# Cluster ties through a triangular matmul, and a new order of loads, moves and lots ahead of the first attention head

## The reference, cut to what matters

```python
def _attn_ref(q, k, v, centroids):                 # q, k, v: 2 x 8 x 768 x 64; centroids: 8 x 16 x 64
    scale = 1.0 / np.sqrt(D)
    q_n, k_n, c_n = ...                            # each row over its norm + 1e-06
    q_assign = np.argmax(np.einsum('bhsd,hcd->bhsc', q_n, c_n), axis=-1)
    k_assign = np.argmax(np.einsum('bhsd,hcd->bhsc', k_n, c_n), axis=-1)
    mask = q_assign[:, :, :, None] == k_assign[:, :, None, :]
    scores = scale * np.matmul(q, k.transpose(0, 1, 3, 2))
    scores = np.where(mask, scores, -1000000000.0)
    scores = scores - np.max(scores, axis=-1, keepdims=True)
    attn = np.exp(scores)
    attn = attn / (np.sum(attn, axis=-1, keepdims=True) + 1e-09)
    return np.matmul(attn, v).astype(np.float32)
...
x = attention, 1536 tokens x 512
h = x @ w_in;   x = (h / (1 + exp(-1.702 * h))) @ w_out              # 512 -> 2048 -> 512
h = x @ w_in2;  s = h * softmax(h)                                   # 512 -> 1024
out = ((s - mean(s)) / sqrt(var(s) + 1e-06) * g_ln) @ w_out2         # 1024 -> 512
```

## Time and profile before

| | |
|---|---|
| median of 3 runs | 666.93 us |
| the profiled execution, its own time | 669.46 us |
| its span, first to last instruction | 667.6 us |
| PE busy | 630.4 us, 94% |
| DVE, POOL, ACT busy | 471.6, 451.9, 354.4 us |
| first matmul of the scores of turn 0 | 34.29 us |
| first `turn` | 46.62 us |
| first matmul of the scores of turn 1 | 61.80 us |

### The profile page before, as it was taken

How to read it: one execution, slowest core, us unless ns; L and a number is a source line. 1 busy time by engine, 2 the same in 40 slices (tenths; PEclk the granted TensorE clock), 3 DMA queues, 4 the chain that set the end, 5 groups by cost and what they waited for, 6 DMA issues and landing times.

```text
span 667.6 us, 11191 instructions
## 1 busy us (share of the span) xinstructions
PE 630.4 (94%) x3245; PEld 529.9 (79%) x3245; DVE 471.6 (71%) x805; ACT 354.4 (53%) x705; POOL 451.9 (68%) x588
## 2 busy tenths in 40 slices
PE   4478999999999999999999999999999999999998
PEld 1267888988989898888878888878888888788876
DVE  3668999999999995564645684855457478778660
ACT  1258989999999985333325344443332144443241
POOL 2667697887988877766675777776666776867100
PEclk9969999999999999999999999999999999999999
DMA  8775545445545340222222222222220000000001
GB/s 279 199 228 138 145 106 144 129 110 143 137 106 145 91 172 32 94 94 96 94 95 94 92 93 97 94 94 93 95 95 32 1 0 17 32 11 23 31 33 47
DMA packets 26937, 64.31 MB, mean 96 GB/s; under 512 B 3872, under 2 KB 10016, under 8 KB 26912
## 3 DMA queue, kind: packets, MB, share of 16 engines
q1 hardware_dynamic: 24896, 60.09, 30.2%
q10 hardware_dynamic: 2016, 3.93, 1.6%
HBM read 46.60 MB, written 4.72 MB: 77 GB/s over the span
## 4 chain that ended last, share of the span: by engine, by line
PE 67%; ACT 10%; issue 7%; DVE 6%; DMA 4%; POOL 4%; DVEq 1%; SPq 1%; ACTq 0%; POOLq 0%
PE banks L581 7%; PE banks L583 7%; PE banks L582 7%; PE banks L596 6%; PE banks L566 6%; PE banks L598 6%; PE banks L597 6%; ACT probs L815 4%; PE banks L551 4%; ACT probs_th L826 3%; PE banks L721 2%; PE banks L720 2%; PE banks L719 2%; ACT x_sums L832 2%; PE banks L690 2%
## 5 line engine op out<-in xcount | busy, mean ns | idle before, releaser
L1065 DVE TENSOR_TENSOR probs_tl<-banks,probs_th 128x384 fp32r<-128x384 f32 x192 | 100.4, 546 | 12.1 <-ACT probs_th L826 9.7
L1045 DVE TENSOR_REDUCE neg_max<-banks 128x1 f32<-128x768 f32 x96 | 91.1, 949 | 9.9 <-PE banks L538 8.0
L826 ACT CAST probs_th<-banks 128x384 fp32r<-128x384 f32 x192 | 83.0, 485 | 22.2 <-PE banks L551 20.8
L1359 POOL TENSOR_TENSOR wait_scrap<-half_power 128x1 f32<-128x1 f32 x128 | 26.6, 208 | 97.7 <-PE banks L598 66.9
L815 ACT ACTIVATE probs<-banks,neg_max 128x768 f32<-128x768 f32 x96 | 88.1, 918 | 7.3 <-DVE neg_max L1045 7.2
L1435 POOL TENSOR_SCALAR probs<-probs,row_inv 128x768 f32<-128x768 f32 x96 | 87.5, 912 | 0.0
L1039 DVE TENSOR_TENSOR gl<-gate,gh 128x512 fp32r<-128x512 f32 x48 | 40.3, 840 | 63.4 <-ACT gh L800 63.4
L551 PE MATMUL banks<-ident,probs 128*128 128x128 f32 x576 | 79.0, 272 | 1.3 <-ACT hot_t L762 1.3
L566 PE MATMUL banks<-probs_th,v_parts 128*128 128x384 f32 x192 | 70.3, 366 | 9.9 <-DVE x_sums L1072 9.9
L1418 POOL TENSOR_TENSOR downl<-gelu_raw,downh 128x512 fp32r<-128x512 f32 x48 | 75.9, 1582 | 4.0
L596 PE MATMUL banks<-gh,downh 128*128 128x512 f32 x192 | 76.1, 396 | 0.4 <-POOL downl L1418 0.2
(11 more groups left out here) (145 smaller groups left out, 1431.9 us busy)
## 6 DMA issues: line engine op xcount, KB each, us to landing
gelu_raw<-w_gelu SPq DMA_DIRECT2D x48, 512.0 KB, 3.2
ln_raw<-w_ln SPq DMA_DIRECT2D x8, 512.0 KB, 4.8
pair_t<-q_t SPq DMA_DIRECT2D x4, 768.0 KB, 8.0
pair_t<-k_t SPq DMA_DIRECT2D x4, 768.0 KB, 9.4
kq_raw<-k_t SPq DMA_DIRECT2D x16, 192.0 KB, 3.6
kq_raw<-q_t SPq DMA_DIRECT2D x16, 192.0 KB, 3.8
q_parts<-k_high SPq DMA_DIRECT2D x16, 192.0 KB, 2.6
q_high<-k_high SPq DMA_DIRECT2D x16, 192.0 KB, 3.0
```

The costliest lines, as they stand in the source:

```text
L826: nc.scalar.copy(probs_th[half % 2][:, c * CH:(c + 1) * CH, i * P:(i + 1) * P], pt_bank(n, c).rearrange("p (t s) -> p t s", t=CH)).then_in ...
L1045: nc.vector.tensor_reduce(out=neg_max[:, col], in_=scores[n % 2], op=ALU.max, axis=mybir.AxisListType.XY, negate=True).then_inc(max_done, 1)
L1065: nc.vector.tensor_tensor(probs_tl[half % 2][at], pt_bank(n, c).rearrange("p (t s) -> p t s", t=CH), probs_th[half % 2][at].bitcast(F32), ...
```

## The change

- Ties are no longer broken by ranks. `compare` gives 1 where a similarity is at its maximum; `ties_of` transposes that (3 transposes a lot), ACT copies it (`copy_ties`), and one matmul with a 128x128 matrix (`first_w`) subtracts from each cluster's mark the marks of the earlier ones of its head; DVE makes `hot_t` from the result with one operation (`choose`), in PSUM to SBUF. Two matrices are built by POOL at the start (`first_weights`). `rank_lot`, the maximum over ranks, `hots_of` and `store_clusters` are gone.
- `hot_t` has four buffers, so both heads of turn 0 take their cluster rows from it, and SP issues all four stores of `mask_rows`, behind head 1's moves.
- On SP, k and q of head 0 are loaded behind lot 1, and head 0's first three moves stand ahead of lots 4 to 7; k and q of head 1 and lots 4 and 5 stand between its moves; the load of the gains comes later.
- Lots 5 (the end), 6 and 7 are worked on inside steps 0 to 5 of turn 0, by a table of steps.
- On PE 52 transposes of the identity onto itself are added: 16 at the start, 6, 8, 6, 6 between lots (`keep_warm`), and 16 right ahead of the first scores. Nobody reads their result.

```diff
-        KQ_STEP, STORE_STEPS, HOT_STEPS, CHOOSE_STEPS = 0, (2, 4), (3, 5), (0, 1)
+        SIMS_STEP = {6: 1, 7: 3}
+        TOKENS_STEP = {6: 2, 7: 4}
+        TIES_STEP = {5: 0, 6: 4, 7: 5}
+        COPY_TIES_STEP = {5: 0, 6: 4, 7: 4}
+        FIRST_STEP = {5: 1, 6: 4, 7: 5}
+        COMPARE_STEP = {6: 3, 7: 4}
+        CHOOSE_STEP = {5: 1, 6: 4, 7: 5}
...
@@ place_head on SP
+                if isinstance(it, int) and it == 0 and j == 0:
+                    load_kq(0, 1)
+                    load_pairs(4)
                 sp.wait_ge(high_moved[j], (it + 1) * 32)
                 move(k_high[j][high, :], k_high[j][low, :], qk_ready[j])
+                if isinstance(it, int) and it == 0 and j == 0:
+                    load_pairs(5)
...
@@ tensor
+            def ties_of(e):
+                pe.wait_ge(compared, e + 1)
+                if e >= 1:
+                    pe.wait_ge(ties_t_copied, e)
+                for i in range(CH):
+                    last = nc.tensor.transpose(ties_ps[:, i * P:(i + 1) * P], ties[e % 2][:, i * P:(i + 1) * P],
+                                               ident[:])
+                last.then_inc(ties_done, 1)
+            def first_of(e):
+                x = e // 2 % 2
+                pe.wait_ge(ties_t_copied, e + 1)
...
+                nc.tensor.matmul(first_ps, first_w[x][:], ties_t[e % 2][:], start=True, stop=True
+                                 ).then_inc(first_done, 1)
+            def keep_warm(turns):
+                for i in range(turns):
+                    nc.tensor.transpose(banks[:, 3, HALF:BANK], ident[:], ident[:])
...
@@ vector
-                nc.vector.tensor_reduce(out=most[:], in_=ranks, op=ALU.max, axis=AX_X).then_inc(rank_max_done, 1)
...
+                nc.vector.tensor_scalar(hot_t[b][x][:, c * HALF:(c + 1) * HALF], first_ps, float(x), -FAR if x else 1.0,
+                                        ALU.is_ge, ALU.mult).then_inc(hot_t_done, 1)
```

More of the change, by code:

```diff
@@ L470, in _ @@
         def _(pe):
-            pe.wait_ge(gpsimd_consts, 4)
+            pe.wait_ge(gpsimd_consts, 3)
+            for i in range(16):
+                nc.tensor.transpose(banks[:, 6, HALF:BANK], ident[:], ident[:])
             pe.wait_ge(cent_unit_done, 1)
@@ new lines, in _ @@
+            sims_of(0)
+            keep_warm(6)
+            tokens_of(0)
+            for e in range(1, 4):
+                sims_of(e)
+                ties_of(e - 1)
+                tokens_of(e)
+                first_of(e - 1)
+            keep_warm(8)
+            ties_of(3)
+            keep_warm(6)
+            first_of(3)
+            sims_of(4)
+            keep_warm(6)
+            tokens_of(4)
+            sims_of(5)
+            ties_of(4)
+            tokens_of(5)
+            first_of(4)
@@ L641, in attention_turn @@
                             head_half(*lagged(it, n, lag, STEPS), c)
+                    for e in range(5, LOTS):
+                        if first and SIMS_STEP.get(e) == n:
+                            sims_of(e)
+                        if first and TIES_STEP[e] == n:
+                            ties_of(e)
+                        if first and TOKENS_STEP.get(e + 1) == n:
+                            tokens_of(e + 1)
+                        if first and FIRST_STEP[e] == n:
+                            first_of(e)
                     if drain and n in UP_STEPS:
@@ L1017, in choose @@
[L1017 to L1030 removed]
+                b, x, c = e // 4, e // 2 % 2, e % 2
@@ L1080, in attention_turn @@
                         row_max(it, n)
-                    if isinstance(it, int) and it == 0 and n in CHOOSE_STEPS:
-                        choose(LOTS - len(CHOOSE_STEPS) + CHOOSE_STEPS.index(n))
+                    for e in range(5, LOTS):
+                        if isinstance(it, int) and it == 0 and CHOOSE_STEP[e] == n:
+                            choose(e)
+                        if isinstance(it, int) and it == 0 and COMPARE_STEP.get(e) == n:
+                            compare(e)
                     if pair:
```

218 lines of the change are left out of this document (102 added, 116 removed).

## The result

The changed kernel takes 669.51 us (median of 8 runs, 668.48 to 670.26), the kernel before 666.96 on the same chip (8 runs, 665.76 to 667.88): ratio 1.0037, 95% interval 1.0026 to 1.0048. So the change makes it 2.5 us slower, where 665.6 was predicted, with 663.6 to 669.0 as the range.

The account below looks back on a forecast made before the run. The start was taken as the bound, through DMAs. First score 3.9 us sooner, 3.6 given back in turn 0; first score of turn 1 from 61.80 to 60.5, so 666.93 - 1.3 = 665.6 us; range 663.6 to 669.0.

Parts of the forecast that it names:

- T1: First score of turn 1, at 61.80 before and predicted at 60.5; whatever moves it moves the end by as much.
- rival 4: Nothing reaches the end: turn 1 may take its pace from ACT and DVE, giving 666.9; chance 0.04.
- the sum's baseline: Runs lie 2.5 below the profiled execution of 669.46, so the gain of 1.3 is taken from 666.93: 665.6.
- Lots 4 and 5: Queue count at the start: lot 4 usable at 23.1, lot 5 at 26.3, with 0.6 for the queue's laggards.
- rival 1: Queue lags as for lot 7: lot 5 usable at 28 to 29.3, time 667.3 to 668.6; chance 0.20.
- From lot 5 to the first score: Lot 5's work, lot 4's matmul and 16 identities on PE: 4.1 us, first score at 30.4 against 34.29.
- The clock should hold: PE's clock stays up through lots 4 and 5, its gaps being 2.1 and 1.1 us against 4.50 before.
- rival 2: PE's clock falls to 0.50 from lot 4 on, costing 4.4, of which about 3.5 stay: 669.1; chance 0.12.
- From the first score to the first turn: Turn 0's steps with two and a half lots in them: 15.9 us against 12.3, first turn at 46.3.
- 3.6 of the 3.9 us are given back: Most of the gain at the first score is lost in turn 0: first turn at 46.3 against 46.62.
- POOL's chain: Of three chains after the first turn the last: k_low of turn 1 ready at 52.8, then 7.7 to 60.5.
- The rule on the shared port pair: By the rule k_low falls from 2.59 to 2 x 1.01, first score up to 0.5 sooner; not in the sum.

Follow-up runs that it names:

- b_again: The kernel before, unchanged, profiled and timed once more: 665.9 us, ratio 0.9989 to the kernel before.
- lots_first: Changed kernel with lots 4 and 5 loaded right behind lot 3, ahead of head 0's moves, and head 1's loads behind head 0's cluster rows: 662.46 us.
- a_fill: Changed kernel with 36 more identity turns on PE between lot 3's triangular matmul and lot 4: 668.5 us, ratio 1.0023 to the kernel before.
- warm_turn0: Changed kernel with 19 more identity turns on PE inside turn 0, useful work in the same order: 668.65 us, ratio 1.0029 to the kernel before.
- ties_alone: Nearly the kernel before plus the triangular matmul, four hot_t buffers and later mask stores; only lot 7's ties and choice inside turn 0, no identities: 662.28 us.
- steps_later: Changed kernel with lot 6's triangular matmul and choose moved from step 4 to step 5: 666.04 us, ratio 0.9994 to the kernel before.
- both: Changed kernel with the edits of lots_first and steps_later together: 662.4 us, ratio 0.9932 to the kernel before.
- ties_lot7: ties_alone with lot 7's load issued ahead of head 0's moves instead of between them: 662.45 us, ratio 0.9923 to the kernel before.
- a_no_warm: Changed kernel without any added identity turn on PE, those at the start included: 668.28 us, ratio 1.0028 to the kernel before.
- both_idle: The kernel of both without any added identity turn on PE: 663.15 us, ratio 0.9939 to the kernel before.

## Why the prediction was wrong, point by point

**Right.** The place: only the start moved, and T1 carried it to the end (rival 4 is out). No wait for `qk_ready` stood behind the identities, and these were on the path. PE's clock went up early through the 16 turns and nobody got the gain. From first score to first `turn` 15.9 was predicted and 16.3 measured, from there to T1 14.2 and 13.6. The first of these agreements is in part luck: the sum has the clock at 1.00 throughout, and it was 0.50 from 43.5 us on, which cost about 0.9. `choose` took 0.55 to 0.56 where 0.5 was set.

**The step that failed: the sum's baseline.** "The runs shown lie 2.5 below the profiled execution's time: 666.93 - 1.3 = 665.6." Two things can't both hold: that the first score gains 3.9 us against 34.29, and that the kernel after lies 2.5 below its own profile just as before. The 34.29 contained the late lot 7 of one execution; `b_again` has 32.05. The profile after lies 0.1 below its median, that of before 2.5 above. Taken from the level 669.46, the error in own time is small: T1 came 1.9 late (1.3 from lot 5, 0.8 from there to the first score, 0.4 up to the first `turn`, 0.6 back up to T1), of which 0.7 came back behind T1, so that 668.2 was predicted and 669.38 measured, 1.2 us. The other 2.7 us are this shift: 665.6 + 1.2 + 2.7 = 669.5. Set against the undisturbed T1 of 58.30 or about 59.3, the predicted T1 of 60.5 is a loss of 1.2 to 2.2 us and no gain of 1.3. The text saw lot 7's 8.5 us and used it as a rival's evidence, but did not ask whether the same event had made the profile long.

**Lots 4 and 5.** 23.1 and 26.3 predicted, 23.75 and 27.59 measured: 1.3 for lot 5, which puts it right at the point where rival 1 began to decide (27.6). 0.65 of it is lot 4's delay already. The sum had lots at 375 GB/s even between moves; the rate was 164 to 332 GB/s from 17 to 25 us. `lots_first` shows that the place in the queue was the matter.

**From lot 5 to the first score.** 4.1 predicted, 4.9 measured. "The clock should hold" failed: PE's gap ahead of lot 4 was 4.49 rather than 2.1, since PE was done with lot 3 at 19.3 rather than 20.9 and lot 4 came 0.65 later, and the granted clock was 0.50 from 23.1 to 29.9. That is rival 2's mechanism, in two falls instead of one and below its price of 3.5: with the clock up over these lots (`a_fill`) the first score came 1.3 us earlier, T1 0.15 in its profile and the median 0.9, not clear of noise; the fall within turn 0 took about 1.8 up to T1 by the profile of `warm_turn0` and 0.5 by its median. Together with lot 5, the first score came at 32.45 rather than 30.4: rivals 1 and 2 in part, both at once.

**From the first score to the first turn.** The number was right, the comparison was with 12.3, and the note that "3.6 of the 3.9 us are given back" was the warning. Against `b_again` nothing is gained before, so this stretch is the whole loss: 16.3 - 12.1 = 4.2 us, with 0.4 more at the first score, of which 0.5 come back up to T1 and 0.7 behind it: 3.4 of span. The medians show 2.5, since `b_again` is 1.0 quicker than the median of 666.96. It is not the price of breaking ties by matmul (`ties_alone` takes 10.9) but of two and a half lots within the steps. `steps_later` takes 2.6 us of it away with one `choose`: about 1.7 by the order and 0.9 by the clock.

**To T1.** POOL's chain was named as last; measured is no wait at all, PE's own chain being last, which was the earliest of the three in the prediction (13.2 behind the first `turn`, 13.6 measured). The stores of `mask_rows` cost nothing here, and become a bound only when turn 0 is shorter (`both`).

**The rule on the shared port pair.** The row of `k_low`:

```profile
12.37 1.96 POOL L1421 TENSOR_TENSOR k_low<-kq_raw,k_high 128x384 fp32r<-128x384 f32 x2 [0.95 <-ACT k_high L819]
```

It took 1.96 instead of 2.59; the sum went by 2.59. The Trainium skill, "SBUF — State Buffer", section "SBUF: two separate sides", has a DVE instruction with two SBUF inputs and a GpSimd instruction that reads SBUF block each other, and without such a DVE instruction the row's undisturbed duration, 2 x 1.01, was to be expected. The trace agrees with it; no run takes this one thing away by itself. The 0.6 us saved did not reach the first score, since lot 5 was last.

## What to carry to other kernels

Compare the profiled execution's own time with the median before anything is summed: when it lies well above, look for the event that made it so, and don't count the removal of that event as a gain. Where one queue feeds two consumers at the start, the order of its DMAs can decide more than the work on the engines (6.5 us here): put the loads that all later work hangs on in one uninterrupted row. Before work is spread over the steps of a pipelined loop, follow it through the in-order lists of all engines: one operation that waited, ahead of one that could run, cost about 1.7 us here. And when filler is added to test a clock, look whether it stands on the path before the difference is read as the clock's price.

## What the runs showed of the hardware that was not expected

- The same kernel's lot 7 was usable at 30.22 in one execution and at 28.06 in another, with T1 3.5 us apart; 35 timed runs of before spread over 664.48 to 669.81, so such an execution is at the edge of what the kernel does.
- A DMA of 192 KB behind lots took long to land: 9.26 us for the move of `k_low` in `ties_lot7` and 9.5 in `ties_alone`, where the earlier trace rows had 7.19, in the first with 1 us at 0 GB/s shortly before.
- The granted clock held at 1.00 over all of turn 0 in `warm_turn0`, and that shortened the stretch from first score to first `turn` by 0.4 us, 0.9 with the added turns on the path taken off, since PE waited on ACT and DVE for most of it.
- Without any identity PE still came to full speed, only later: a lot's similarities took 1.51 us at 9.09 and 0.85 from 12.37 on in `a_no_warm` (9.41 and 12.79 in `both_idle`), where after has 0.85 from 6.69 on, and the time was no worse than with them. The clock column of the windows reads 1.00 over all of this, the 1.51 included; this early in the span the durations tell the clock and the column does not.
